# Prefix scan first in both passes of an attention recurrence, and m2 moved ahead of the state's last product

## The chip, the cores and the metric

One core of a Trainium2 chip. The metric is the device time of one execution in microseconds, here the median of several runs. The kernel computes a recurrent attention followed by two expert layers. The change touches the attention alone.

## The reference, cut to what matters

The attention keeps a 40 x 40 state for each of 32 heads (4 batches x 8) over 768 time steps:

```python
for t in range(S):
    y[:, :, t] = einsum('bhd,bhde->bhe', r_t, state)
    Sa = einsum('bhde,bhe->bhd', state, a_t)
    state = state * w_t[:, :, None, :] - einsum('bhd,bhe->bhde', Sa, b_t) \
            + einsum('bhd,bhe->bhde', v_t, k_t)
```

Its output goes through a router that picks one of 8 experts for each token (`_moe_ref`) and a dense layer (`_moe2_ref`). Both stay as they are.

## The kernel before, in words

Time is cut into 12 chunks of 64 steps. The partitions hold two heads in halves of 64, 40 rows of each in use; the free dimension holds 8 slots (`HS`) of 64 times. Two halves of the batch run one after the other, so there are `STEPS` = 24 chunk steps in each pass.

**Decays as scans.** Within a chunk the decay from one time to another is a product of w. VectorE computes it with two `tensor_tensor_scan` operations over one row of 8 x 66 elements (`WIDE` = 66: a pad of zero at either end of each slot): `suffixes` (L433) scans backward and starts at 1, `prefix_starts` (L440) takes the reciprocal of the total into `restart`, `prefixes` (L444) scans forward and starts at 1 / total. `scaled_second` (L452) multiplies b (or k) by the suffixes, `scaled_alpha` (L455) multiplies a by the prefixes. In the second pass `prefixes` also copies the total from `suf` into column 65 of `wq` (L450).

**First pass** (L486 to L505 on VectorE, L685 on ScalarE, L905 on TensorE): for each chunk the products of alpha with second (g1) and the turned second (bt). ScalarE evicts them, SyncE stores g1's blocks to DRAM and loads them again for the inversion, which VectorE does for two groups of chunks and GpSimd for the four others (`invert_blocks`, up to about 292 us). One step runs at the pace of VectorE's five operations. TensorE waits for alpha, the last of them, and SyncE's load of the chunk three ahead into the ring `t_in` waits for it too (`s_alpha1`).

**Second pass** (L512 on VectorE, L745 on ScalarE, L932 on TensorE): one turn for each chunk, and in each turn TensorE works through eighteen groups of 32 small matmuls (`heads`), each of which may wait for an eviction. The order in each engine's queue is written out by hand. The end of a turn on TensorE before the change is: sa's product (L955), sat's product (L956), the part of y from rr and st (L957), the last part of the state (sa with btm, did "st", L959), m2's product (rr with sat, L961), g2's product of the next chunk (L963), `picks` (L965, of the previous chunk's output, waits for `out_of["st"]`), and y's last product (L967, waits for the masked m2). In the trace these groups are, in that order, bank<-w_tm,inv; inv,w_tm; rr,st; sa_tm,btm; rr,sat; alpha,second; pick,yt; m,btm.

ScalarE evicts sa (L758) and then sat (L760). VectorE scales the next state by the total of the *next* chunk (`swt`, L550), taken from column 65 of `wq` and from its crossed copy, and then masks m2 (L554). The crossed copy is made by two DMAs from SyncE, `cross_wq` (L339), in front of the load of t_in (L383), the store of rows (L385) and the loads of vtm, vt, inverses and rr. `y_out` (L458) scales y by the prefixes.

Of the kernel before, what the change touches and what calls it, by code (L numbers as in the profile page):

```python
# [10 lines left out]
ALU = mybir.AluOpType  # L11
# [4 lines left out]
PARTS = 128  # L16
BATCH, HEADS, SEQ, DIM = 4, 8, 768, 40
HALF = PARTS // 2
C = 64
# [141 lines left out]
def attention(nc, inp, dram, keep):  # L161

    with ExitStack() as ctx:
# [32 lines left out]
        def late_part(n, **sizes):  # L196
# [41 lines left out]
        s_set, s_suf, s_rw, s_wq, s_wc, s_second, s_alpha1, s_alpha0, s_alpha = (m_.sem(n) for n in (  # L238
            "s_set", "s_suf", "s_rw", "s_wq", "s_wc", "s_second", "s_alpha1", "s_alpha0", "s_alpha"))
# [31 lines left out]
        def _(sp):  # L271
            def load_t(j):
                if j >= TR:
                    if j - TR < STEPS:
                        sp.wait_ge(s_alpha1, j - TR + 1)
                    elif j - TR == STEPS:
                        sp.wait_ge(s_alpha0, 1)
                    else:
                        sp.wait_ge(s_second, j - TR + 1)
# [59 lines left out]
            def cross_wq(k):  # L339
                sp.wait_ge(s_wc, k + 1)  # L340
                if k >= 3:
                    sp.wait_ge(out_of["y"], k - 1)
# [61 lines left out]
        def _(dve):  # L404
# [4 lines left out]
            dve.memset(restart[:, :, WIDE - 1:WIDE], 1.0).then_inc(s_set, 1)  # L409
# [22 lines left out]

            def suffixes(j):  # L433
                dve.wait_ge(s_t[j % TR], 16 * (j // TR + 1))
# [5 lines left out]
            def prefix_starts(j):  # L440
                dve.wait_ge(s_suf, j + 1)
                dve.reciprocal(restart[:, :, 0:1], suf[j % 2][:, :, 1:2]).then_inc(s_rw, 1)

            def prefixes(j):  # L444
                dve.wait_ge(s_rw, j + 1)
                dve.tensor_tensor_scan(out=forward(wq[j % 3][:, :, :]), data0=forward(w_of(j)), data1=forward(restart[:, :, :]), initial=0.0,
                                       op0=ALU.mult, op1=ALU.add).then_inc(s_wq, 1)
                dve.wait_ge(s_wq, j + 1)
                if j >= STEPS:
                    dve.tensor_copy(wq[j % 3][:, :, WIDE - 1:WIDE], suf[j % 2][:, :, 1:2]).then_inc(s_wc, 1)  # L450

            def scaled_second(j):  # L452
                dve.tensor_tensor(second[:, :, :], in_of(j, 1), suf[j % 2][:, :, 2:WIDE], ALU.mult).then_inc(s_second, 1)

            def scaled_alpha(j, sem):  # L455
                dve.tensor_tensor(alpha[:, :, :], in_of(j, 0), wq[j % 3][:, :, 0:C], ALU.mult).then_inc(sem, 1)  # L456
# [29 lines left out]
            for k in range(STEPS):  # L486
                suffixes(k)
                prefix_starts(k)
                prefixes(k)
                if k >= 1:  # L490
                    dve.wait_ge(did["bt"], k)
# [1105 lines left out]
```

## Time and profile before

| | us |
|---|---|
| median of 3 runs | 1057.15 (1055.74 to 1058.28) |
| the profiled execution | 1054.7 |
| its span | 1052.9 |
| TensorE busy | 952.9 (90%) |
| VectorE busy | 711.5 (68%) |
| ScalarE busy | 442.8 (42%) |
| GpSimd busy | 268.6 (26%) |

Shares over the whole span mix stages with different limits. Attention ends near 373 us; its first pass ends near 133 us. Starts and durations in a timeline are in us from the span's start; the ends of matmuls are modelled, and a group "x32" is one call of `heads`. The time from the start of one group to the start of the next is what the group costs the queue.

### The profile page before, as it was taken

Reading aid. Unit: us, or ns where it says so; the run is one execution under the profiler, and the core shown is the slowest. Engines: PE = TensorE matmul, PEld = TensorE weight load, DVE = VectorE, ACT = ScalarE, POOL = GpSimd, SP = SyncE. Lnnn points to the kernel's source line nnn. Section 1 sums busy time; section 2 is a strip of 40 time slices with the busy share of each in tenths; the row PEclk is TensorE's granted clock in tenths of the full one; section 3 lists DMA queues with packets and bytes.
Section 4 is the critical chain, followed back from the end, with each engine's and each line's share of the span. In section 5 each row is a group of like instructions: output and inputs, shape, how many; then the busy total and the mean of one; then the engine's idle time right before and its main releaser. Section 6 shows DMA issues by size and latency. Waiting matters only on the chain. (4 is left out here: it accounts for less than half of the span.)

```text
span 1052.9 us, 48691 instructions
## 1 busy us (share of the span) xinstructions
PE 952.9 (90%) x21425; PEld 874.8 (83%) x21425; DVE 711.5 (68%) x1076; ACT 442.8 (42%) x940; POOL 268.6 (26%) x348
## 2 busy tenths in 40 slices
PE   3526779999999998999999999879999999999997
PEld 2426769999999958998999999668999999999997
DVE  8997958899988764555555555567666565656664
ACT  5525635755555604545555555513222212222211
POOL 1009989798900003222111100241001000000000
PEclk9999988999999999999999999999999999999999
DMA  7968866898898539998676755120100101010100
GB/s 220 234 173 189 203 140 188 242 246 236 238 243 241 150 119 307 332 294 278 190 249 214 228 169 169 41 79 13 38 1 26 26 1 26 2 26 1 26 1 26
DMA packets 116866, 153.19 MB, mean 145 GB/s; under 512 B 68516, under 2 KB 87860, under 8 KB 116420
## 3 DMA queue, kind: packets, MB, share of 16 engines
q1 hardware_dynamic: 102468, 118.68, 40.3%
q0 software_dynamic: 5872, 25.28, 7.8%
q10 hardware_dynamic: 8464, 8.43, 2.4%
q8 instruction: 36, 0.59, 0.2%
q14 instruction: 26, 0.21, 0.1%
HBM read 126.72 MB, written 19.23 MB: 139 GB/s over the span
## 5 line engine op out<-in xcount | busy, mean ns | idle before, releaser
L1468 ACT CAST g_hi<-g 128x512 fp32r<-128x512 f32 x96 | 59.5, 620 | 278.0 <-DVE g L1412 274.4
L1321 PE MATMUL y_bank<-w_out_hi,g_hi 128*128 128x320 f32 x380 | 119.0, 313 | 5.1 <-DVE g_lo L1386 4.3
L1109 PE MATMUL h_bank<-xt,w 128*128 128x128 f32 x992 | 122.0, 282 | 1.8 <-issue 1.8
L1149 DVE TENSOR_TENSOR w_lo<-w_all,w_hi 128x640 fp32r<-128x640 f32 x124 | 101.7, 826 | 31.9 <-ACT w_hi L1189 27.0
L1109 PEld LDWEIGHTS h_bank<-xt,w 128*128 128x128 f32 x992 | 115.8, 195 | 6.0 <-issue 2.2
L1321 PE MATMUL y_bank<-w_out_hi,g_lo 128*128 128x320 f32 x380 | 118.0, 310 | 0.0
L1321 PE MATMUL y_bank<-w_out_lo,g_hi 128*128 128x320 f32 x380 | 117.9, 310 | 0.0
L1408 DVE TENSOR_SCALAR neg<-h_bank,slope 128x512 f32<-128x512 f32 x96 | 72.0, 750 | 65.8 <-PE h_bank L1308 65.4
L1308 PE MATMUL h_bank<-xt_hi,w_in_hi 128*128 128x512 f32 x288 | 113.1, 393 | 0.5 <-DVE xt_hi L1369 0.5
L1308 PE MATMUL h_bank<-xt_hi,w_in_lo 128*128 128x512 f32 x288 | 112.1, 389 | 0.0
L1386 DVE TENSOR_TENSOR g_lo<-g,g_hi 128x512 fp32r<-128x512 f32 x96 | 66.5, 693 | 65.9 <-ACT g_hi L1468 64.5
L1142 DVE SCALAR_TENSOR_TENSOR ht_lo<-h_bank,ht_hi 128x512 fp32r<-128x512 f32 x62 | 42.8, 692 | 88.6 <-ACT ht_hi L1182 83.7
L1189 ACT CAST w_hi<-w_all 128x640 fp32r x124 | 89.7, 727 | 29.3 <-PE y_bank L1121 20.6
L127 POOL TENSOR_TENSOR solved<-solved,share 128x31 f32<-128x31 f32 (+15 forms) x124 | 99.2, 800 | 9.7
L784 PE MATMUL bank<-alpha,second 40*64 40x64 f32 x1568 | 44.6, 269 | 56.5 <-DVE alpha L456 55.7
L124 POOL TENSOR_TENSOR share<-solved,blk 128x31 f32<-128x31 f32 (+15 forms) x124 | 89.0, 718 | 9.7
L784 PEld LDWEIGHTS bank<-alpha,second 40*64 40x64 f32 x1568 | 38.6, 178 | 59.8 <-issue 59.8
L95 POOL DMA_INDIRECT x<-x_rows_mid,order x31 | 32.1, 1035 | 197.8 <-DVE order L609 97.5
L1321 PEld LDWEIGHTS y_bank<-w_out_hi,g_hi 128*128 128x128 f32 x380 | 71.9, 189 | 10.6 <-DVE g_lo L1386 5.9
L1121 PE MATMUL y_bank<-w_hi,ht_hi 128*128 128x320 f32 x248 | 79.2, 319 | 0.0
L1182 ACT ACTIVATE ht_hi<-h_bank 128x512 fp32r<-128x512 f32 x62 | 37.1, 598 | 97.3 <-PE h_bank L1109 97.3
L1121 PE MATMUL y_bank<-w_lo,ht_hi 128*128 128x320 f32 x248 | 76.7, 309 | 0.0
(213 smaller groups left out, 2145.1 us busy)
## 6 DMA issues: line engine op xcount, KB each, us to landing
w<-w_in SPq DMA_DIRECT2D x31, 1024.0 KB
t_in<-wak_in SPq DMA_DIRECT2D x24, 679.0 KB, 5.7
t_in<-wab_in SPq DMA_DIRECT2D x21, 679.0 KB, 5.0
w_all<-w_in POOLq DMA_DIRECT2D x8, 1280.0 KB, 9.2
rr<-rr_in SPq DMA_DIRECT2D x24, 336.0 KB, 3.5
w_rest<-w_in SPq DMA_DIRECT2D x62, 128.0 KB
vtm<-vtm_in SPq DMA_DIRECT2D x24, 240.0 KB, 3.7
vt<-vt_in SPq DMA_DIRECT2D x24, 224.0 KB, 4.0
```

The lines of the kernel that those rows point to most:

```text
L124: link(eng.tensor_tensor(part, q[:, 0:j + 1, j:j + 1].to_broadcast(shape), h[:, j:j + 1, j + 1:B].to_broadcast(shape), ALU.mult))
L127: link(eng.tensor_tensor(rest, rest, part, ALU.subtract))
L784: last = pe.matmul(out[HALF * to:HALF * to + rows_out, row, n * i:n * i + n], lhs, rhs, start=opens and i == 0, stop=closes and i == HP - 1)
L1109: last = pe.matmul(h_bank[s][h][:, f * ET:(f + 1) * ET], w1[s][:, k, (FH * h + f) * PARTS:(FH * h + f + 1) * PARTS], xt[s][:, k, :], start ...
L1121: last = pe.matmul(y_bank[s][:, 0:FEAT], h[s][:, f, :], w[:, f, :], start=f == 0 and n == 0, stop=f == NF - 1 and n == 2)
L1149: dve.tensor_tensor(piece(w2_lo, p), of_expert(e, p), piece(w2_hi, p).bitcast(F32), ALU.subtract).then_inc(s_w2lo, 1)
L1189: act.copy(piece(w2_hi, p), of_expert(e, p)).then_inc(s_w2hi, 1)
L1308: last = pe.matmul(h_bank[j % 2][:, :], w[:, k, f * PARTS:(f + 1) * PARTS], x_part[b % 2][:, k, :], start=n == 0, stop=n == len(passes) - 1)
L1321: last = pe.matmul(y_bank[n][:, 0:FEAT], g_part[j % RING][:, n * PARTS:(n + 1) * PARTS], v[:, f, :], start=f == 0 and p == 0, stop=f == NF ...
L1386: dve.tensor_tensor(g_lo[j % RING][:, :], g[j % 2][:, :], g_hi[j % RING][:, :].bitcast(F32), ALU.subtract).then_inc(s_glo, 1)
L1408: dve.tensor_scalar(neg[j % 2][:, :], h_bank[j % 2][:, :], 0.0, keep.slope[:, f:f + 1], ALU.min, ALU.mult).then_inc(s_neg, 1)
L1468: act.copy(g_hi[j % RING][:, :], g[j % 2][:, :]).then_inc(s_ghi, 1)
```

## The change

- `prefixes` runs first and starts at 1, so column 64 of `wq` holds the total; `suffix_starts` takes its reciprocal into the other end of `restart`; `suffixes` runs last and starts at 1 / total. The copy of the total into column 65 is gone, and the wait of the second scan on itself with it.
- `scaled_alpha` comes ahead of `scaled_second` in the first pass; TensorE and SyncE's loads wait for `s_second`.
- In the second pass the prefix scan stands where the suffix scan was and the other way round. The state is scaled at the end of a chunk by that chunk's own total.
- `cross_wq(k)` waits for the prefix scan instead of the copy, and for the output of one chunk later, from k = 2 on.
- ScalarE evicts sat ahead of sa. TensorE computes sat ahead of sa, and m2 ahead of the last product of the state. VectorE masks m2 ahead of the scaling of the state.

```diff
--- before.py
+++ after.py
@@ -235,8 +235,8 @@
         s_blk, s_tt = ([[m_.sem(f"{n}{s}_{part}") for part in range(GROUP)] for s in range(3)] for n in ("s_blk", "s_tt"))
         s_ax_vtm, s_vt_rr = (m_.sem(n) for n in ("s_ax_vtm", "s_vt_rr"))
         s_step, s_step_dve = m_.sem("s_step"), m_.sem("s_step_dve")
-        s_set, s_suf, s_rw, s_wq, s_wc, s_second, s_alpha1, s_alpha0, s_alpha = (m_.sem(n) for n in (
-            "s_set", "s_suf", "s_rw", "s_wq", "s_wc", "s_second", "s_alpha1", "s_alpha0", "s_alpha"))
+        s_set, s_suf, s_rw, s_wq, s_second, s_alpha0, s_alpha = (m_.sem(n) for n in (
+            "s_set", "s_suf", "s_rw", "s_wq", "s_second", "s_alpha0", "s_alpha"))
         names = ("turned", "across", "joint", "g1", "bt", "w", "s", "u", "ktm", "z", "m1", "sa", "sat", "st", "g2", "m2", "y", "pick")
         did = {n: m_.sem("pe_" + n) for n in names}
         out_of = {n: m_.sem("ev_" + n) for n in names}
@@ -271,12 +271,7 @@
         def _(sp):
             def load_t(j):
                 if j >= TR:
-                    if j - TR < STEPS:
-                        sp.wait_ge(s_alpha1, j - TR + 1)
-                    elif j - TR == STEPS:
-                        sp.wait_ge(s_alpha0, 1)
-                    else:
-                        sp.wait_ge(s_second, j - TR + 1)
+                    sp.wait_ge(s_second, j - TR + 1)
                 src = inp["wab"][j] if j < STEPS else inp["wak"][j - STEPS]
                 used = slice(0, PARTS if j < TR else USED)
                 sp.dma_start(t_in[j % TR][used, :], src[used]).then_inc(s_t[j % TR], 16)
@@ -337,9 +332,9 @@
                 sp.dma_start(vt[0:USED], inp["vt"][k][0:USED]).then_inc(s_vt_rr, 16)
 
             def cross_wq(k):
-                sp.wait_ge(s_wc, k + 1)
-                if k >= 3:
-                    sp.wait_ge(out_of["y"], k - 1)
+                sp.wait_ge(s_wq, STEPS + k + 1)
+                if k >= 2:
+                    sp.wait_ge(out_of["y"], k)
                 at = wq_both[(STEPS + k) % 3]
                 for h in two:
                     sp.dma_start(at[rows(h), HS:HS + HP, :], at[rows(1 - h), HP:HS, :]).then_inc(s_wqx[k % 2], 16)
@@ -406,7 +401,7 @@
             dve.memset(keep.eye[:, :], 0.0).then_inc(s_ones, 1)
             dve.memset(restart[:, :, :], 0.0).then_inc(s_set, 1)
             dve.wait_ge(s_set, 1)
-            dve.memset(restart[:, :, WIDE - 1:WIDE], 1.0).then_inc(s_set, 1)
+            dve.memset(restart[:, :, 0:1], 1.0).then_inc(s_set, 1)
             dve.memset(swt[:, :, :], 0.0).then_inc(out_of["st"], 1)
             dve.memset(yt[:, :, :], 0.0)
             dve.wait_ge(s_const, 4)
@@ -430,30 +425,30 @@
             def own_and_crossed(k, part):
                 return wq_both[(STEPS + k) % 3][:, :, part].rearrange("q (g p) t -> q g p t", p=HP)[:, 0:3:2]
 
+            def prefixes(j):
+                dve.wait_ge(s_t[j % TR], 16 * (j // TR + 1))
+                if j >= 1:
+                    dve.wait_ge(s_suf, j)
+                dve.tensor_tensor_scan(out=forward(wq[j % 3][:, :, :]), data0=forward(w_of(j)), data1=forward(restart[:, :, :]), initial=0.0,
+                                       op0=ALU.mult, op1=ALU.add).then_inc(s_wq, 1)
+
+            def suffix_starts(j):
+                dve.wait_ge(s_wq, j + 1)
+                dve.reciprocal(restart[:, :, WIDE - 1:WIDE], wq[j % 3][:, :, C:C + 1]).then_inc(s_rw, 1)
+
             def suffixes(j):
-                dve.wait_ge(s_t[j % TR], 16 * (j // TR + 1))
+                dve.wait_ge(s_rw, j + 1)
                 if j >= 2:
                     dve.wait_ge(s_second, j - 1)
                 dve.tensor_tensor_scan(out=backward(suf[j % 2][:, :, :]), data0=backward(w_of(j)), data1=backward(restart[:, :, :]), initial=0.0,
                                        op0=ALU.mult, op1=ALU.add).then_inc(s_suf, 1)
 
-            def prefix_starts(j):
+            def scaled_second(j):
                 dve.wait_ge(s_suf, j + 1)
-                dve.reciprocal(restart[:, :, 0:1], suf[j % 2][:, :, 1:2]).then_inc(s_rw, 1)
-
-            def prefixes(j):
-                dve.wait_ge(s_rw, j + 1)
-                dve.tensor_tensor_scan(out=forward(wq[j % 3][:, :, :]), data0=forward(w_of(j)), data1=forward(restart[:, :, :]), initial=0.0,
-                                       op0=ALU.mult, op1=ALU.add).then_inc(s_wq, 1)
-                dve.wait_ge(s_wq, j + 1)
-                if j >= STEPS:
-                    dve.tensor_copy(wq[j % 3][:, :, WIDE - 1:WIDE], suf[j % 2][:, :, 1:2]).then_inc(s_wc, 1)
-
-            def scaled_second(j):
                 dve.tensor_tensor(second[:, :, :], in_of(j, 1), suf[j % 2][:, :, 2:WIDE], ALU.mult).then_inc(s_second, 1)
 
-            def scaled_alpha(j, sem):
-                dve.tensor_tensor(alpha[:, :, :], in_of(j, 0), wq[j % 3][:, :, 0:C], ALU.mult).then_inc(sem, 1)
+            def scaled_alpha(j):
+                return dve.tensor_tensor(alpha[:, :, :], in_of(j, 0), wq[j % 3][:, :, 0:C], ALU.mult)
 
             def y_out(k):
                 dve.wait_ge(did["y"], k + 1)
@@ -484,30 +479,30 @@
                 return dve.tensor_tensor(by_row(dst), wide(src), later, ALU.mult)
 
             for k in range(STEPS):
+                prefixes(k)
+                suffix_starts(k)
                 suffixes(k)
-                prefix_starts(k)
-                prefixes(k)
                 if k >= 1:
                     dve.wait_ge(did["bt"], k)
+                scaled_alpha(k)
                 scaled_second(k)
-                scaled_alpha(k, s_alpha1)
                 if k == AT_DVE:
                     for g in range(BY_DVE):
                         for part in range(GROUP):
                             dve.wait_ge(s_blk[g][part], 16)
                     dve.wait_ge(s_eye, 2)
                     invert_halves(dve, s_step_dve, blk, solved, share_dve)
+            prefixes(STEPS)
+            suffix_starts(STEPS)
             suffixes(STEPS)
-            prefix_starts(STEPS)
-            prefixes(STEPS)
             dve.wait_ge(did["bt"], STEPS)
+            scaled_alpha(STEPS).then_inc(s_alpha0, 1)
             scaled_second(STEPS)
-            scaled_alpha(STEPS, s_alpha0)
-            suffixes(STEPS + 1)
+            prefixes(STEPS + 1)
+            suffix_starts(STEPS + 1)
             dve.wait_ge(did["g2"], 1)
             masked(g2, BC).then_inc(out_of["g2"], 1)
-            prefix_starts(STEPS + 1)
-            prefixes(STEPS + 1)
+            suffixes(STEPS + 1)
             first_choices = chain(dve, s_choice)
             for k in range(STEPS):
                 more = k + 1 < STEPS
@@ -519,13 +514,15 @@
                         dve.sem_inc(out_of["pick"], 1)
                 dve.wait_ge(did["w"], k + 1)
                 if more:
-                    scaled_alpha(STEPS + k + 1, s_alpha)
+                    scaled_alpha(STEPS + k + 1).then_inc(s_alpha, 1)
                 if k + 2 < STEPS:
-                    suffixes(STEPS + k + 2)
+                    if k >= 1:
+                        dve.wait_ge(out_of["y"], k + 1)
+                    prefixes(STEPS + k + 2)
                 dve.wait_ge(did["m1"], k + 1)
                 masked(m1, BB).then_inc(out_of["m1"], 1)
                 if k + 2 < STEPS:
-                    prefix_starts(STEPS + k + 2)
+                    suffix_starts(STEPS + k + 2)
                 dve.wait_ge(did["z"], k + 1)
                 w_flat = w_tm[:, :, :].rearrange("q (r p) e -> q r (p e)", r=2)
                 dve.tensor_tensor(w_flat, w_flat, BA[:, :, 0:HP * DIM], ALU.add).then_inc(out_of["z"], 1)
@@ -535,23 +532,23 @@
                 else:
                     dve.sem_inc(s_second, 1)
                 if k + 2 < STEPS:
-                    prefixes(STEPS + k + 2)
+                    suffixes(STEPS + k + 2)
                 elif k + 2 == STEPS:
                     dve.wait_ge(s_iota, 8)
                     choices_top(FIRST, first_choices)
                 else:
                     dve.memset(one_hot[:, :, FINAL], 0.0)
                     choices_one(FIRST, first_choices).then_inc(s_hot, 1)
+                dve.wait_ge(did["m2"], k + 1)
+                masked(m2, BA).then_inc(out_of["m2"], 1)
                 dve.wait_ge(did["st"], k + 1)
                 if (k + 1) % NCHUNK == 0:
                     last = dve.memset(swt[:, :, :], 0.0)
                 else:
-                    dve.wait_ge(s_wqx[(k + 1) % 2], 32 * turn(k + 1))
+                    dve.wait_ge(s_wqx[k % 2], 32 * turn(k))
                     last = dve.tensor_tensor(by_row(swt), BD[:, :, 0:HP * DIM].rearrange("q r (p e) -> q r p e", e=DIM),
-                                             own_and_crossed(k + 1, slice(WIDE - 1, WIDE)).to_broadcast([PARTS, 2, HP, DIM]), ALU.mult)
+                                             own_and_crossed(k, slice(C, C + 1)).to_broadcast([PARTS, 2, HP, DIM]), ALU.mult)
                 last.then_inc(out_of["st"], 1)
-                dve.wait_ge(did["m2"], k + 1)
-                masked(m2, BA).then_inc(out_of["m2"], 1)
                 if more:
                     dve.wait_ge(did["g2"], k + 2)
                     masked(g2, BC).then_inc(out_of["g2"], 1)
@@ -754,10 +751,10 @@
                 act.copy(btm[:, :, :].rearrange("q p e -> q (p e)"), btm_all[:, k].rearrange("q p e -> q (p e)"))
                 if k + 1 < STEPS:
                     cross_alpha(k + 1)
+                act.wait_ge(did["sat"], k + 1)
+                act.copy(by_row(sat[:, :, :]), wide(BA)).then_inc(out_of["sat"], 1)
                 act.wait_ge(did["sa"], k + 1)
                 act.copy(flat(sa_tm[:, :, :]), narrow(BC)).then_inc(out_of["sa"], 1)
-                act.wait_ge(did["sat"], k + 1)
-                act.copy(by_row(sat[:, :, :]), wide(BA)).then_inc(out_of["sat"], 1)
                 if k + 1 < STEPS:
                     act.wait_ge(did["z"], k + 1)
                     off_diagonal(k + 1)
@@ -892,7 +889,7 @@
                 return lambda b, p: (across_now[quarter(b), p, :], d1_now[s][quarter(b), p, :])
 
             def g1_product(count):
-                arrive(s_alpha1, count)
+                arrive(s_second, count)
                 arrive(out_of["g1"], count)
                 heads(with_alpha(second), BA, C, done="g1")
 
@@ -925,7 +922,7 @@
                 pe.wait_ge(out_of[n], JOINED + 1)
             pe.wait_ge(out_of["bt"], STEPS + 1)
             warm(2)
-            pe.wait_ge(s_alpha0, 1)
+            pe.wait_ge(s_second, STEPS + 1)
             heads(with_alpha(second), BC, C, done="g2")
             warm(3)
             pe.wait_ge(keep.s_gw, 32)
@@ -952,13 +949,13 @@
                 arrive(out_of["m1"], i)
                 heads(from_k(lambda i, q, m: m1[rows(m), slot(q, i), :]), BB, C, closes=False)
                 arrive(out_of["z"], i)
+                heads(sat_product, BA, C, done="sat")
                 heads(sa_product, BC, DIM, done="sa")
-                heads(sat_product, BA, C, done="sat")
                 heads(from_s(lambda i, q, m: at_m(rr, i, q, m, live(m))), BB, C, opens=False, closes=False)
+                arrive(out_of["sat"], i)
+                heads(m2_product, BA, C, done="m2")
                 arrive(out_of["sa"], i)
                 heads(from_b(lambda i, q, m: sa_tm[rows(m), slot(q ^ m, i), :]), BD, DIM, opens=False, done="st")
-                arrive(out_of["sat"], i)
-                heads(m2_product, BA, C, done="m2")
                 arrive(s_second, i + (STEPS + 1))
                 heads(with_alpha(second), BC, C, done="g2")
                 arrive(out_of["st"], i + 1)
```

## Rows read from the trace of the kernel before

**Rows 1.** The page, busy time of each engine over the span.

```profile
PE 952.9 (90%) x21425; PEld 874.8 (83%) x21425; DVE 711.5 (68%) x1076; ACT 442.8 (42%) x940; POOL 268.6 (26%) x348
```

**Rows 2.** Windows: stretch, busy us of each engine, granted clock, DMA share, GB/s.

```profile
25.00:50.00 25.00, 11.67 (x384) 10.96 (x384) 24.30 (x33) 13.28 (x37) 0.00 (x0) 1.00 0.94 240
...
155.00:160.00 5.00, 5.00 (x200) 4.82 (x196) 2.93 (x4) 1.28 (x3) 4.56 (x6) 0.50 0.90 252
...
200.00:225.00 25.00, 23.99 (x1537) 22.84 (x1539) 23.51 (x36) 16.75 (x44) 23.04 (x26) 1.00 0.92 247
...
300.00:350.00 50.00, 48.31 (x3167) 46.05 (x3157) 42.14 (x72) 28.96 (x71) 0.00 (x0) 1.00 0.88 237
```

**Rows 3.** Timeline of VectorE, one first-pass step: start us, us, engine, line, operation.

```profile
21.50 1.25 DVE L437 TENSOR_TENSOR_SCAN suf<-t_in,restart 128x528 f32<-128x528 f32 x1
...
23.03 1.26 DVE L446 TENSOR_TENSOR_SCAN wq<-t_in,restart 128x528 f32<-128x528 f32 x1
24.32 0.69 DVE L453 TENSOR_TENSOR second<-t_in,suf 128x512 f32<-128x512 f32 x1
...
25.53 1.25 DVE L437 TENSOR_TENSOR_SCAN suf<-t_in,restart 128x528 f32<-128x528 f32 x1
```

**Rows 4.** Timeline of VectorE, a contended turn: a scan, what follows it, the copy.

```profile
171.86 1.69 DVE L437 TENSOR_TENSOR_SCAN suf<-t_in,restart 128x528 f32<-128x528 f32 x1
173.47 0.66 DVE L484 TENSOR_TENSOR m<-bank,later 128x512 f32<-128x512 f32 x1
...
176.80 0.39 DVE L450 COPY wq<-suf 128x8 f32<-128x8 f32 x1
```

**Rows 5.** Timeline of VectorE, first pass, the two long waits for TensorE.

```profile
91.83 0.69 DVE L453 TENSOR_TENSOR second<-t_in,suf 128x512 f32<-128x512 f32 x1 [2.09 <-PE bank L784]
...
100.18 0.89 DVE L453 TENSOR_TENSOR second<-t_in,suf 128x512 f32<-128x512 f32 x1 [3.61 <-PE bank L784]
```

**Rows 6.** Timeline of TensorE, end of a quiet turn (matmul groups).

```profile
314.23 0.66 PE L784 MATMUL bank<-w_tm,inv 64*64 64x40 f32 x32
...
316.13 0.69 PE L784 MATMUL bank<-rr,sat 40*64 40x64 f32 x32
316.62 0.68 PE L784 MATMUL bank<-alpha,second 40*64 40x64 f32 x32
317.08 0.66 PE L846 MATMUL bank<-pick,yt 40*64 40x48 f32 x32
317.72 0.66 PE L784 MATMUL bank<-m,btm 64*40 64x64 f32 x32
```

**Rows 7.** Timeline of VectorE in the same turn.

```profile
316.16 0.49 DVE L550 TENSOR_TENSOR swt<-bank,wq 128x320 f32<-128x320 f32 x1
316.88 0.69 DVE L484 TENSOR_TENSOR m<-bank,later 128x512 f32<-128x512 f32 x1 [0.23 <-PE bank L784]
```

**Rows 8.** Timeline of ScalarE in the same turn.

```profile
314.95 0.43 ACT L758 COPY sa_tm<-bank 128x320 f32<-128x320 f32 x1 [1.95 <-PE bank L784]
315.40 0.59 ACT L760 COPY sat<-bank 128x512 f32<-128x512 f32 x1
```

**Rows 9.** Timeline of TensorE, the contended turn with the longest wait for swt.

```profile
270.31 0.68 PE L784 MATMUL bank<-alpha,second 40*64 40x64 f32 x32
271.18 0.68 PE L846 MATMUL bank<-pick,yt 40*64 40x48 f32 x32 [0.19 <-DVE swt L550]
271.78 0.66 PE L784 MATMUL bank<-m,btm 64*40 64x64 f32 x32
```

**Rows 10.** Timeline of SyncE's DMA issues in a quiet turn.

```profile
309.93 0.59 SPq L282 DMA_DIRECT2D t_in<-wak_in  x1
...
313.57 0.35 SPq L332 DMA_DIRECT2D vtm<-vtm_in  x1
```

**Rows 11.** The tile vtm in the second pass: time from issue to landing.

```profile
DMA to landing us min/median/max: 2.6/3.7/5.0
```

**Rows 12.** Timeline of TensorE, a turn that starts late.

```profile
327.85 0.22 PE L784 MATMUL bank<-swt,alpha 40*64 40x40 f32 x1 [0.39 <-DMA vtm<-vtm_in]
```

## The prediction

> **What bounds the kernel now.** I read four views. The busy shares [rows 1] say only that TensorE is the fullest engine over all stages; the windows [rows 2] cut the span where the change acts. In the first pass (from 5 to 133 us) VectorE is the full engine, 24.30 of 25 us, and TensorE is under half. In the second pass (139 to 373 us, 24 turns of one loop) it is TensorE: 48.31 of 50 us at 300 to 350, where GpSimd is silent, and 23.99 of 25 at 200 to 225, where GpSimd inverts blocks and VectorE too stands at 23.51. After 373 us nothing is touched; what attention gains or loses reaches the end whole. The timelines then give each chain.
>
> **First pass.** One step is 4.03 us (21.50 to 25.53 [rows 3]), VectorE's five operations end to end: scan, reciprocal, scan, two products. The change keeps all five but swaps the scans and the products. What goes is one wait that an operation makes on its own engine's last result. Before, the second scan is followed by a wait on itself and `second` starts 0.03 us after its end (23.03 + 1.26 = 24.29, then 24.32 [rows 3]). After, `scaled_alpha` needs only the older scan and follows the suffix scan without waiting; such a follower starts 0.08 us before the end (171.86 + 1.69 = 173.55, then 173.47 [rows 4]). So 0.11 us a step. `second` waits for the suffix scan, but that ends during the alpha product. TensorE's first product waits for the last product of the step as before, SyncE's load waits for `second` in place of `alpha`, again the last. Of the 25 steps, 23 are bound by VectorE; in two it waits 2.09 and 3.61 us for TensorE [rows 5], and there 0.11 us buys nothing. 23 x 0.11 = **2.5 us less**. DMA engines are busy 0.94 of this stretch [rows 2]; at a period of 3.92 that would be 0.97, near the edge, so the gain may be anything between 0 and 2.5. I take 2.5 because in the uncontended steps like the one shown the scan waits for no load.
>
> The Trainium skill, "VectorE: DVE Perf Modes", § The DRAIN you can't avoid, says that chaining operations with or without a semaphore costs the same. By it the 0.11 us would be 0 and the first pass unchanged. Rows 3 and 4 speak against it: 0.03 us after the end with a wait, 0.08 before the end without.
>
> **The copy of the total.** The copy into `wq` goes in 24 places. In the quiet part of the second pass swt's product starts only with TensorE's release (316.16 us [rows 7]), so the copy is covered. In the contended part it takes 0.39 us ahead of swt [rows 4] and is on the way to the picks in the steps where VectorE is late. What takes its place decides what that is worth, next.
>
> **Second pass, TensorE's new order.** I take the quiet step and count from the start of the product that yields `sa` (314.23 [rows 6]), call it 0. Today the picks start at 2.85 and the product that yields y at 3.49 (317.08, 317.72). The picks need swt, y's product needs the masked m2. Today swt is computed first, well before the picks, and m2's mask (316.88 [rows 7]) is what y's product waits for: mask end 317.57, product 317.72, so 0.15 from VectorE's end to TensorE's start.
>
> After the change:
> - sat's product stands at 0 and lasts 0.66 or so [rows 6]; ScalarE takes it 0.06 later and needs 0.59 [rows 8]; TensorE starts 0.14 after that: m2's product at 1.45, against a bare queue time of 1.35. It starts 1.90 today.
> - m2's product ends at 1.45 + 0.69 = 2.14; VectorE's mask starts 0.06 later, 2.20.
> - The mask holds VectorE for 0.61. swt comes **behind it** on VectorE, at 2.81 at the earliest, though st's product (1.94 + 0.52 = 2.46) was ready. 0.49 for swt [rows 7]: 3.30.
> - The picks, behind their wait for swt, start at 3.44 instead of 2.85. Everything on TensorE's queue waits with them.
> - y's product follows after a bare group spacing of 0.48 (316.13 to 316.62 is 0.49, 316.62 to 317.08 is 0.46 [rows 6]), since m2 is long there: 3.92 instead of 3.49.
>
> So a quiet step becomes **0.43 us longer**. The old wait of 0.15 us for m2 goes, and a new one of 0.59 us for swt comes: the state's last product moved back by a whole product, and swt moved back behind the mask too. Downstream (g2's mask, yt, alpha) VectorE has 0.2 us or more of waiting for TensorE and moves along.
>
> There are 8 quiet turns of 9.0 us. Seven cost 0.43; the last has a memset of 0.33 us in place of swt's product and costs 0.27: 3.3 us.
>
> In the 14 turns between 170 and 300 us GpSimd slows VectorE (a scan takes 1.69 us [rows 4] against 1.25), and the picks wait for swt already today by 0 to 0.41 us; the worst turn goes from 270.31 to 271.18 where 0.46 is bare [rows 9]. By the same groups in the timeline of each, the stretch from sa's product to y's is 3.50 to 3.87 us, in sum 50.5. The new stretch is 3.92 in each (3.76 in the one with a memset) as long as the scan ends before m2's product; in the worst turn it ends 2.26 after 0, so an unwaited mask could start at 2.18, just ahead of the 2.20. Sum 54.7: **4.2 us more**. The two first turns, partly at 0.50 of the full clock [rows 2], follow the same logic, about 0.35 each: 0.7. Second pass: 3.3 + 4.2 + 0.7 = **8.2 us more**.
>
> **Queues behind the moved waits.** SyncE's crossing of wq for turn k+1 now waits for y_out(k-1), about 1.4 us later than today; the 679 KB load of t_in behind it (309.93 [rows 10]) goes out near 311.35. Its own reader is a turn further on, so it is covered. But vtm's load, issued at 313.57, now runs right behind it. It takes 3.7 us, at worst 5.0 [rows 11], and the loop's first product needs it at 318.58: one turn already waits 0.39 us for it [rows 12]. The longer turn gives 0.43 back. Bounds: -0.5 (today's waits for vtm vanish) and +0.4 in half of the turns, +4. I take 0. The wait added on VectorE (prefixes on y_out) is met when it is reached, since y_out stands ahead of it in the same queue.
>
> **Sum.** -2.5 + 8.2 = +5.7 us. The profiled execution took 1054.7 us with a span of 1052.9, so it would take 1060.4. The runs' median is 1057.15, 2.5 above it; **1057.15 + 5.7 = 1062.8 us**.
>
> **Rivals.**
> - *Faster: VectorE's relief wins.* In the contended turns VectorE is nearly full [rows 2]; each turn loses a copy and a wait, 0.39 + 0.11 us, and TensorE's waits for VectorE there, 2.0 us in sum at the picks and 2.3 at the masked m1, could vanish. With the first pass, -2.5 - 4.3: 1050.4. It needs swt no later than today, that is the mask of m2 out of its way; that holds only where the scan ends later than m2's product by the mask's 0.6 us, and no turn shows that. Against it also: alpha's start, which the masked m1 hangs on, waits for TensorE. Chance 0.11.
> - *Cancelled.* The mask finds room while the scan runs late in most contended turns, so that these lose only the 0.05 us of the worst one; 3.3 + 0.7 + 0.7 - 2.5: +2.2 us or less, 1057 to 1059.3. Chance 0.12.
> - *First pass gives nothing* (the page's rule, or DMA at 0.94 binding): +8.2, 1065.4. Chance 0.17.
> - *The later t_in costs vtm's readers*: +1 to +4 on top, 1064 to 1067. Chance 0.12.
> - *The clock.* TensorE runs at half its clock at 155 to 160 us [rows 2] after the first turn's pauses. A stretch of that kind that ends sooner or later would move the time by some us either way, whatever the change does; about 0.04 each way, inside the other cases.
> - *The forecast itself*, 1060 to 1064: 0.48.
>
> Within 0.2% is 1055.0 to 1059.3, about what a measurement of this kernel can tell from no change. Faster 0.11, same 0.12, slower 0.77. The range leaves out the faster rival and a few hundredths above: 1056.5 to 1068.
>
> **What the profile would show.** First-pass period 3.92 us, the alpha product starting 0.08 before the suffix scan's end. In a quiet turn: m2's product at 1.45, its mask at 2.20, swt at 2.81, the picks at 3.44 with VectorE's swt as what TensorE waited for in nearly all turns, no wait for m, a period of 9.44. Wrong if the picks start by 2.9, if the quiet period stays at 9.0, if waits for vtm are many, or if the first pass keeps 4.03.

## The result, and the profile after

The changed kernel takes 1066.87 us in the median of 4 runs (1065.77 to 1069.86), the kernel before 1056.45 (1054.51 to 1058.28, 4 runs): ratio **1.0111, 95% interval 1.0087 to 1.0136**. Beside other kernels on another chip it was 1.0136 (1.0095 to 1.0177). Slower, as forecast, but by 10.4 us where 5.7 were forecast, at the upper edge of the range.

The profiled execution after has a span of 1068.1 us, 15.2 above that before; it was the longest of its four. One profile below, that of e1, is of a slow execution (1064.47 us at a mean granted clock of 0.975; that kernel's fastest took 1048.06), so no size is taken from it. The difference by stage, from the timelines of TensorE (start of a turn = first product of swt with alpha):

| stretch | before, us | after, us | difference | forecast |
|---|---|---|---|---|
| to the start of turn 0 | 139.04 | 136.64 | -2.4 | -2.5 |
| turns 0 and 1 | 30.68 | 32.00 | +1.3 | +0.7 |
| turns 2 to 22 (21 turns) | 194.42 | 208.77 | +14.35 | +7.2 |
| turn 23 and all behind | 688.8 | 690.7 | +1.9 | +0.3 |

The last line is mostly not the change's: that stretch took 683 to 694 us in the fourteen profiles of this study, whatever was done to attention; turns 0 and 1, partly at half the clock, took 27 to 33, so the +1.3 of the second line is inside that spread too (the changed kernel's other profile, e12, has 30.0 us there, 0.7 less than before). Single runs of one kernel spread by 10 us or more, so the size of each term below is read from the timelines. What needs an explanation is the third line. First the end of a quiet turn after the change, TensorE and then VectorE, to be set against [rows 6] and [rows 7]:

```profile
322.83 0.65 PE L781 MATMUL bank<-inv,w_tm 64*40 64x64 f32 x32
323.28 0.65 PE L781 MATMUL bank<-w_tm,inv 64*64 64x40 f32 x32
323.72 0.66 PE L781 MATMUL bank<-rr,st 40*40 40x64 f32 x32
324.26 0.69 PE L781 MATMUL bank<-rr,sat 40*64 40x64 f32 x32
324.75 0.51 PE L781 MATMUL bank<-sa_tm,btm 64*40 64x40 f32 x32
325.19 0.69 PE L781 MATMUL bank<-alpha,second 40*64 40x64 f32 x32
326.25 0.68 PE L843 MATMUL bank<-pick,yt 40*64 40x48 f32 x32 [0.36 <-DVE swt L549]
326.73 0.66 PE L781 MATMUL bank<-m,btm 64*40 64x64 f32 x32
327.68 0.22 PE L781 MATMUL bank<-swt,alpha 40*64 40x40 f32 x1 [0.30 <-issue]
```

```profile
325.02 0.69 DVE L479 TENSOR_TENSOR m<-bank,later 128x512 f32<-128x512 f32 x1 [0.57 <-PE bank L781]
325.62 0.48 DVE L549 TENSOR_TENSOR swt<-bank,wq 128x320 f32<-128x320 f32 x1
```

From sat's product at 322.83: m2's product at 1.43 us, its mask at 2.19, swt at 2.79, the picks at 3.42, y's product at 3.90. The forecast had 1.45, 2.20, 2.81, 3.44 and 3.92. That mechanism is there as it was worked out, in nearly every turn. Three things were not worked out. The first is the last row: the next turn starts 0.95 us after y's product. Before, from the last row of [rows 6] at 317.72 to this one, it was 0.86:

```profile
318.58 0.22 PE L784 MATMUL bank<-swt,alpha 40*64 40x40 f32 x1 [0.20 <-issue]
```

The second is in the list of what TensorE waited for, all turns from the third on (operation waited with, us in total, times, longest):

```profile
PE bank L843 <- DVE swt L549: 7.3, 20, 0.4
...
PE bank L781 <- DMA rr<-rr_in: 3.3, 5, 1.3
PE bank L781 <- DMA vtm<-vtm_in: 3.0, 6, 0.9
```

and the same list of before:

```profile
PE bank L784 <- DVE m L484: 0.9, 4, 0.3
PE bank L784 <- DMA vtm<-vtm_in: 0.8, 2, 0.4
PE bank L846 <- DVE swt L550: 0.2, 1, 0.2
```

The waits for swt were forecast. The waits for two loads, 6.3 us of idle TensorE against 0.8, were not. One of them in the timeline, m1's product held 0.66 us for the load of rr and vt:

```profile
339.46 0.68 PE L781 MATMUL bank<-w_tm,inv 64*64 64x40 f32 x32
340.80 0.69 PE L781 MATMUL bank<-rr,vt 40*64 40x64 f32 x32 [0.66 <-DMA rr<-rr_in]
```

SyncE's issues show where these loads come from; in [rows 10] t_in went out 3.64 us ahead of vtm, now it is 2.37:

```profile
318.66 1.11 SPq L340 DMA_DIRECT2D wq<-wq  x2
319.81 0.61 SPq L277 DMA_DIRECT2D t_in<-wak_in  x1
...
322.18 0.35 SPq L327 DMA_DIRECT2D vtm<-vtm_in  x1
...
325.01 0.33 SPq L322 DMA_DIRECT2D rr<-rr_in  x1
```

Counted from the start of the turn, t_in goes out at 1.67 us in the median, 0.33 before: 1.3 us later. vtm goes out at the same 4.0 us, but its landing went from 3.7 us (median, [rows 11]) to 4.8.

The third is TensorE's clock. In turn 6 of the changed kernel (turns are counted from 0) TensorE waited 0.93 us for vtm and then 1.32 for rr, and behind the second wait the granted clock fell to its lower level, 0.50 (1.2 GHz of 2.4), for 3.4 us. The two waits and the clock before, in and behind that stretch:

```profile
208.37 0.22 PE L781 MATMUL bank<-swt,alpha 40*64 40x40 f32 x1 [0.93 <-DMA vtm<-vtm_in]
...
212.13 0.69 PE L781 MATMUL bank<-rr,vt 40*64 40x64 f32 x32 [1.32 <-DMA rr<-rr_in]
```

```profile
207.50:213.70 6.20, 4.02 (x260) 3.86 (x261) 4.39 (x6) 2.60 (x7) 5.65 (x8) 1.00 0.95 218
213.70:217.10 3.40, 3.40 (x148) 3.40 (x148) 2.75 (x3) 0.67 (x2) 3.17 (x4) 0.50 0.97 262
217.10:221.00 3.90, 3.24 (x205) 2.98 (x201) 2.19 (x4) 3.76 (x11) 3.51 (x6) 1.00 0.61 152
```

The late products of that turn took 4.75 us where the turns around it took 3.9. In turns 2 to 22 of the kernel before the clock was 1.00 throughout.

To compare kernels I add up, over turns 2 to 22, from the starts of TensorE's groups: the **order** stretch (first late product to y's product), the time of u's group over its bare 0.57 us (**held for rr and vt**), the **gap** from y's product to the next turn at its smallest, what its sum has above that (mostly **held for vtm**), and how long the clock was at its **lower level** in these turns. One profile stands behind each row; the two of the changed kernel agree within 0.7 us over the 21 turns, and so do those of e5 and e6. All in us:

| kernel | 21 turns | order stretch, mean | held for rr, vt | smallest gap | above it | lower clock |
|---|---|---|---|---|---|---|
| before | 194.4 | 3.57 | 0.6 | 0.85 | 0.7 | 0 |
| changed | 208.8 | 3.94 | 4.9 | 0.95 | 1.5 | 3.4 |
| changed, again (e12) | 208.1 | 3.92 | 4.8 | 0.95 | 0.7 | 3.4 |
| order only (e2) | 203.6 | 3.99 | 0.0 | 0.95 | 0.4 | 0 |
| late load only (e11) | 204.3 | 3.66 | 7.2 | 0.85 | 2.8 | 6.8 |
| scans and late load (e1) | 206.9 | 3.62 | 6.4 | 0.85 | 5.7 | 13.7 |
| changed, swt ahead (e4) | 206.2 | 3.78 | 5.2 | 0.85 | 3.0 | 6.8 |
| changed, load first (e3) | 201.4 | 3.90 | 0.0 | 0.95 | 0.4 | 0 |
| changed, three semaphores (e8) | 202.2 | 3.90 | 0.0 | 0.95 | 0.4 | 0 |
| scans, load first (e5) | 195.8 | 3.50 | 5.3 | 0.85 | 0.8 | 0 |
| e5 and a wait in the first pass (e6) | 195.8 | 3.51 | 3.6 | 0.85 | 1.4 | 0 |
| scans, three semaphores (e7) | 192.5 | 3.50 | 1.6 | 0.85 | 1.0 | 0 |
| e7, sat first (e9) | 196.7 | 3.67 | 1.7 | 0.85 | 0.5 | 0 |
| e7, m2 first (e10) | 206.1 | 4.21 | 0.0 | 0.85 | 0.4 | 0 |

So the 14.35 us of the changed kernel are 21 x 0.37 = 7.7 of order, 4.3 held for rr and vt, 0.8 for vtm, 21 x 0.10 = 2.1 of gap, and -0.5 of the rest. About 0.8 of the 7.7 is the one turn at the lower clock: where the changed order runs with its loads in time (e3, e8) it is 6.9.

The last column goes with the late load. In each of the five profiles that have it (changed, e12, e11, e1, e4) the clock fell in these turns, each time behind waits for vtm or rr in the same turn (0.34 and 1.13 us in e12; 0.74 and 1.21, then 0.51 and 1.37 in e11; 0.52 and 1.14, then 2.11 in e1; 1.84 in e4); in the other nine it never fell. Such waits don't always bring it: in turn 4 of e5 TensorE waited 0.34 and then 1.36 us, and the clock stayed at 1.00.

### The profile page after: what moved, and what is told of

The parts are those of the page before. It is cut to its first block and busy times, and to the rows that moved or that the text cites. A ratio compares the mean times of both kernels' runs of the same rounds, so it can differ in the third digit from the quotient of the medians.

```text
span 1068.1 us, 48716 instructions
## 1 busy us (share of the span) xinstructions
PE 953.7 (89%) x21425; PEld 876.1 (82%) x21425; DVE 701.3 (66%) x1052; ACT 440.6 (41%) x940; POOL 265.8 (25%) x348
## 5 line engine op out<-in xcount | busy, mean ns | idle before, releaser
L127 POOL TENSOR_TENSOR solved<-solved,share 128x31 f32<-128x31 f32 (+15 forms) x124 | 95.6, 771 | 9.7
## 6 DMA issues: line engine op xcount, KB each, us to landing
w_all<-w_in POOLq DMA_DIRECT2D x8, 1280.0 KB, 10.2
```

Source lines behind the costliest of these rows:

```text
L127: link(eng.tensor_tensor(rest, rest, part, ALU.subtract))
```

## The experiments

Theory A: the new order makes the picks late. Theory C: the crossing of wq, and with it the load of t_in, go out later, and that costs TensorE waits for the loads behind it. Rival B to A: the late load is what costs, the order little.

**e2, the order alone.** The kernel before with only the swaps on TensorE, ScalarE and VectorE:

```diff
+                heads(sat_product, BA, C, done="sat")
                 heads(sa_product, BC, DIM, done="sa")
-                heads(sat_product, BA, C, done="sat")
...
+                arrive(out_of["sat"], i)
+                heads(m2_product, BA, C, done="m2")
                 arrive(out_of["sa"], i)
...
-                arrive(out_of["sat"], i)
-                heads(m2_product, BA, C, done="m2")
```

> The kernel before with only the new order at the end of a turn (sat ahead of sa, m2 ahead of the state's last product, m2's mask ahead of swt). Scans, copy and SyncE's waits are those of before. Theory A: picks at 3.44 us after the turn's first late product, sum 8 to 10 us on top of before, 1064 to 1067, and no more waits for rr and vtm than before. Rival B: under 3 us on top of before.

Measured: ratio 1.0072 (1.0038 to 1.0106), 1058.36 us beside 1050.48 for the kernel before on that chip. The 21 turns take 9.1 us more, the loads hold nobody. Theory A holds. The order stretch gives 8.8 of the 9.1 us, more than the 7.2 forecast; what is more lies in the contended turns (up to 4.29 us, against 3.89 in the quiet ones). The gap gives 2.1, and 1.8 comes back, half of it from the loads that hold nobody now.

**e1, all but the order.** The changed kernel with the four swaps undone.

> The changed kernel with the old order at the end of a turn: sa ahead of sat on TensorE and ScalarE, the state's last product ahead of m2, swt ahead of m2's mask. The scans, the missing copy and SyncE's later waits stay. Theory A (the order costs the time: picks 0.59 us late in each turn): the turn's end returns to 3.49 us from sa's product to y's, so 9 us less than the changed kernel's 1067, 1054 to 1058. Rival B (the later load of t_in costs most): waits for rr and vtm stay, and the time stays above 1061.

Measured: ratio 1.0052 (1.0011 to 1.0093), 1058.07 us beside 1050.48. The order stretch is back (3.62), and yet the 21 turns took 206.9 us. In the profiled execution TensorE waited 6.9 us for vtm and 4.4 for rr, and behind the longest of these waits, 2.1 us, the clock was at its lower level from 285.9 to 296.1 us, so the 12.5 us over before are no measure of the late load:

```profile
PE bank L781 <- DMA vtm<-vtm_in: 6.9, 8, 2.1
PE bank L781 <- DMA rr<-rr_in: 4.4, 8, 1.1
```

The expected 1054 to 1058 was counted from a kernel before of 1056.45; beside the 1050.48 of this chip it is 1048 to 1052. Theory A fell as the whole cause: what is left without the order costs too.

**e11, the late load alone.** The kernel before with one condition changed:

```diff
-                if k >= 3:
-                    sp.wait_ge(out_of["y"], k - 1)
+                if k >= 2:
+                    sp.wait_ge(out_of["y"], k)
```

> The kernel before with one line changed: the crossing of wq waits for the output of one chunk later, as in the change, so that it and the load of t_in behind it go out some 1.4 us later. Theory C (the late load costs by itself, and more where the turn is short): waits for vtm and rr of 8 us or more in the 21 turns from turn 2, which take over 202 us in place of 194.4; 6 to 10 us slower than before. Rival (the late load hurts only beside the new order or the new scans): under 197 us for these turns and no measurable change.

Measured: ratio 1.0080 (1.0048 to 1.0112), and in the turns 9.9 us more, of which 6.6 are waits for rr and vt and 2.1 for vtm; another 2.2 us are the order stretches of the two turns at the lower clock (4.69 and 4.48 where 3.50 is usual). The waits of TensorE:

```profile
PE bank L784 <- DMA rr<-rr_in: 5.3, 9, 1.4
PE bank L784 <- DMA vtm<-vtm_in: 4.0, 8, 0.7
```

vtm's load takes 4.7 us to land instead of 3.7:

```profile
DMA to landing us min/median/max: 2.6/4.7/5.6
```

One condition on SyncE costs 9.9 us in the turns where the whole change costs 14.35. With the changed order the same late load costs less, 6.5 to 7.4 us by e8 and e3 below; that this is because each turn is longer already is my reading.

**e3 and e8, the changed kernel with the load in time.** e3 puts the load ahead of the crossing:

```diff
-                if more:
-                    cross_wq(k + 1)
                 if k + TR < STEPS:
                     load_t(STEPS + k + TR)
+                if more:
+                    cross_wq(k + 1)
```

> The changed kernel with SyncE's load of t_in issued ahead of the crossing of wq, so that it no longer stands behind the wait for y_out. Theory C (the later load is what came on top of the forecast): the waits for rr and vtm, 6.3 us in sum, go back to under 1.5, and the time falls by 4 to 6 us to 1061 to 1063. Rival: these waits come from the longer turn itself or from the crossing, and the time stays within 1 us of 1067.

e8 gives the crossings three semaphores in turn instead of two. With two, the crossing of chunk k+1 must not count up a semaphore on which y_out(k-1) still waits; with three, it only has to wait for y_out(k-2), as before the change:

```diff
+        s_wqx = [m_.sem(f"s_wqx{s}") for s in range(3)]
...
-                if k >= 2:
-                    sp.wait_ge(out_of["y"], k)
+                if k >= 3:
+                    sp.wait_ge(out_of["y"], k - 1)
...
-                    dve.wait_ge(s_wqx[k % 2], 32 * turn(k))
+                    dve.wait_ge(s_wqx[k % 3], 32 * turn(k, 3))
```

> The changed kernel whole, with three semaphores for the crossings, so that crossing and load go out where they did before. Theory C (late load): turns as in the run with the load ahead of the crossing, 201 us from turn 2 to the last (changed kernel: 208.8), no wait for rr or vtm; 6 to 7 us under the changed kernel. Rival (it was the crossing, or having the load ahead of everything, that helped there): 205 us or more.

Measured: e3 1.0070 (1.0030 to 1.0109), e8 1.0075 (1.0042 to 1.0109); 201.4 and 202.2 us for the 21 turns, 7.4 and 6.5 less than the changed kernel, and no wait for a load in either, nor a lower clock. Both agree with theory C: 5 of these us are the time held for rr and vt, about 1 that for vtm, 0.8 the slow late products of turn 6. The totals say less. e3 was expected 4.6 to 6.6 us over the kernel before and came 8.9 over the one on its chip, and both intervals overlap that of the changed kernel. What is left over before, 7.0 and 7.8 us, is the order with its gap less what the scans give (against e7, which has the scans and the old order, e8 takes 9.7 us more). e8's list of waits holds these and no load:

```profile
PE bank L844 <- DVE swt L550: 6.9, 19, 0.4
...
PE bank L782 <- DVE m L480: 0.8, 3, 0.3
```

**e4, swt ahead of the mask on VectorE,** the rest as changed.

> The changed kernel with swt ahead of m2's mask on VectorE; TensorE's order stays new. If VectorE's queue (the mask in front of swt) is half of the delay, swt starts 2.52 us after the first late product and the picks at 3.16 instead of 3.43; y's product then waits for the mask, 3.75 instead of 3.91: 3 to 4 us less in sum, 1063 to 1064. If only TensorE's order matters, no change from 1067.

Measured: 1.0087 (1.0052 to 1.0122). In a quiet turn:

```profile
338.61 0.64 PE L781 MATMUL bank<-inv,w_tm 64*40 64x64 f32 x32
...
341.75 0.68 PE L843 MATMUL bank<-pick,yt 40*64 40x48 f32 x32
342.35 0.66 PE L781 MATMUL bank<-m,btm 64*40 64x64 f32 x32
```

The picks start 3.14 us after the first late product and y's product 3.74, as expected (3.16, 3.75). So of the 0.57 us by which the picks came late, 0.28 was VectorE's queue (the mask in front of swt) and the rest TensorE's (the state's last product moved back). The order stretch falls by 0.16 us a turn. 3 to 4 us less were expected; the 21 turns take 2.6 less, and the total shows no clear gain. Waits for vtm grow (3.0 above the smallest gap), and behind one of them, 1.84 us, the clock was at its lower level for 6.8 us: that turn took 12.1 us where 9.3 is usual.

**e9 and e10, the two swaps one by one,** on the kernel of e7 below.

> The kernel with the scans and three semaphores, and of the new order only sat ahead of sa (TensorE and ScalarE). Expected in a quiet turn: the state's last product at 1.81 us after the first late product instead of 1.35 (it waits for sa's copy behind sat's), picks at 3.2, y's product at 3.85. It also tells whether the longer gap at the loop's end (0.95 instead of 0.86 us) comes with this swap.

> The kernel with the scans and three semaphores, and of the new order only m2's product ahead of the state's last product, with sa still ahead of sat and swt ahead of the mask. Expected in a quiet turn: m2 waits for sat's copy, 1.90 instead of 1.35; picks at 3.6, y's product at 4.2, as far behind as the mask waits for swt. It also tells whether the longer gap at the loop's end comes with this swap.

e9: a single run, 1053.31 us. The group ahead of the state's last product takes 0.87 us where 0.45 is bare, and 0.22 of the 0.43 comes back behind it, since m2's product is no longer held for sat's copy. y's product comes at 3.67 in the mean, not 3.85: 0.17 us a turn over e7. e10: a single run, 1061.96 us, m2's product held for sat's copy (the group ahead of it takes 1.00), y's product at 4.21, as expected. Moving m2 ahead is the dear part, unless sat goes ahead too. Neither alone shows the gap of 0.95.

**The gap.** The smallest gap is 0.95 us in the kernels where y's product is not held for m2's mask (changed, e2, e3, e8, e12) and 0.85 in all where it is (before, e1, e4, e5, e6, e7, e9, e10, e11). So of the 0.15 us that the old wait for m2 cost in front of y's product, 0.10 had been covering something at the loop's end that is now bare. That the sequencer catches up during that wait is my reading; it was not tested by itself.

**e5 and e6, the scans, and a wait that isn't needed.** e5 is e1 with the load first. e6 adds one line to it, in the first pass:

```diff
                 if k >= 1:
                     dve.wait_ge(did["bt"], k)
+                dve.wait_ge(s_suf, k + 1)
                 scaled_alpha(k)
```

> The scans of the change (prefix first, no copy), the old order at the end of a turn, and the load of t_in ahead of the crossing. If the scans and the missing copy are worth what the rows say: 3.3 us in the first pass (0.15 us in 22 steps) and up to 2 us in the turns in which GpSimd is busy: 1051 to 1053, faster than before by 0.4%. If the scans bring nothing outside the first pass: 1053 to 1054.

> The same kernel with one wait added in each first-pass step: the alpha product waits for the suffix scan in front of it on the same engine, which it doesn't need. If such a wait costs a start at the end of the scan instead of before it: 0.11 to 0.15 us in each of some 22 steps, 2.5 to 3.4 us more than the kernel without it. By the page of the Trainium skill on VectorE, where a semaphore between two operations costs nothing: no difference.

Measured: e5 0.9991 (0.9963 to 1.0018), e6 1.0010 (0.9977 to 1.0044). The totals can't tell them apart; the timelines of VectorE can. e5 and then e6, a first-pass step:

```profile
22.49 1.26 DVE L443 TENSOR_TENSOR_SCAN suf<-t_in,restart 128x528 f32<-128x528 f32 x1
23.66 0.67 DVE L451 TENSOR_TENSOR alpha<-t_in,wq 128x512 f32<-128x512 f32 x1
...
24.85 1.25 DVE L432 TENSOR_TENSOR_SCAN wq<-t_in,restart 128x528 f32<-128x528 f32 x1
```

```profile
23.22 1.26 DVE L443 TENSOR_TENSOR_SCAN suf<-t_in,restart 128x528 f32<-128x528 f32 x1
24.58 0.69 DVE L451 TENSOR_TENSOR alpha<-t_in,wq 128x512 f32<-128x512 f32 x1
...
25.80 1.25 DVE L432 TENSOR_TENSOR_SCAN wq<-t_in,restart 128x528 f32<-128x528 f32 x1
```

Without the wait the alpha product starts 1.17 us after the scan, with it 1.36, and the step takes 3.89 against 4.10 us in each of the first steps. The Trainium skill, "VectorE: DVE Perf Modes", § The DRAIN you can't avoid, says of eight copies in a row that a semaphore after each costs nothing extra. Here one costs 0.2 us behind a scan of 1.26, so the measurement decides against it for this pair of operations.

Where GpSimd is active the same wait costs nothing. The periods of the steps from about 105 us on are 5.27, 5.33, 5.27, 5.21, 5.03 us in e6 and 5.28, 5.33, 5.25, 5.17, 5.03 in e5. The alpha product starts 0.10 to 0.11 us after the scan's end in the one and 0.07 to 0.09 before it in the other, but it then lasts 0.83 to 0.89 against 1.03 to 1.10 us.

e5 missed its 1051 to 1053: with the load *ahead* of everything, m1's product was held 4.0 us for rr in three of the early turns:

```profile
PE bank L781 <- DMA rr<-rr_in: 4.0, 3, 1.6
```

Earlier is not simply better either. Beside the new order, whose turns are longer, the same placing caused no wait (e3).

**e7, the best of it.** The scans of the change, the old order, and the three semaphores, so that crossing and load go out as before.

> The scans of the change, the old order at the end of a turn, and three semaphores for the crossings of wq in place of two, so that a crossing (and the load of t_in behind it) needs no wait for the newest y_out and goes out where it did before. If the late load was the whole extra cost and the scans bring what the first pass showed: waits for rr and vtm as before (u's group 0.57 to 0.60 us a turn), 24 turns in no more time than before (second turn to last under 194 us), 2 us less at the end of the first pass, and a time 0.2 to 0.5% under that of before. Rival: the scans disturb the loads in another way, and the waits stay.

Measured: 1050.82 us beside 1054.78, ratio **0.9945 (0.9917 to 0.9973)**: faster than the kernel before, by 0.5%. The 21 turns take 192.5 us; the picks never wait for swt (mean spacing 0.47 us against 0.56 before).

**e12** is the changed kernel once more, beside e11.

> The changed kernel as it is, beside the run above on the same chip: by the first measurement 1.1% over the kernel before, with 3 to 7 us of waits for rr and vtm in the 21 turns from turn 2. It shows how far these waits repeat from one execution to another.

Measured: ratio 1.0136 (1.0095 to 1.0177). Its waits repeat: 3.2 us for rr and 1.9 for vtm, and in turn 6 the clock fell for 3.4 us again, behind waits of 0.34 and 1.13 us.

## Why the forecast was half right

**The order, 8.2 us forecast.** Right in mechanism and nearly in size. Each number of the quiet turn came within 0.02 us. In 21 turns it was 7.7 us against 7.2, of which about 0.8 belongs to the lower clock of one turn. The 0.7 for the first two turns can't be judged: +1.3 in one profile, -0.7 in the other. That the picks wait for VectorE's swt in nearly every turn shows (20 times, 7.3 us of idle time), and there is no wait for the masked m2 any more.

**"... and +0.4 in half of the turns, +4. I take 0."** This is the step that failed, the term of the sum for the queues behind the moved waits. The forecast saw that t_in would go out 1.4 us later and that vtm ran behind it, then reasoned from one load and its median landing time. The runs show 5.1 us held for loads in the 21 turns, and it was mostly the other one: rr and vt, which m1's product needs, 4.3 us. Putting the load back in time takes 6.5 (e8) to 7.4 us (e3) out of the changed kernel, the lower clock behind the waits included, so that is what the term measured where 0 was taken. e11 shows it in the kernel before: 9.9 us. The queue as a whole had to be weighed: DMA engines 0.88 busy there [rows 2], and t_in and six more transfers in one queue behind a wait that now ends 1.3 us later in a turn of 9 us. By which of them the delay reaches rr and vt no run takes apart. The rival for it was there, with 0.12 and a price of 1 to 4; the price was too low. The rival on the clock took such a stretch for independent of the change; here it came with the waits for loads.

The 5.7 us forecast, the late load and the gap below make 14 to 15 us. That fits the changed kernel beside e11 (14.7 us between medians) and the two profiled executions (15.2), and is above the 10.4 of the first medians, whose interval reaches to 14.4.

**The gap, not in the forecast.** "The old wait of 0.15 us for m2 goes" was counted as a full gain inside the 3.92. 0.10 of it came back at the loop's end, 2.1 us in 21 turns; a quiet turn that no load holds takes 9.50 us, not 9.44. Why it comes back is open.

**First pass, -2.5 forecast, -2.4 found at the start of turn 0,** by other parts than written, so that the two agree is partly luck. The quiet steps gave 0.14 us, not 0.11 (3.89 against 4.03; 15 steps, 2.1 us). The six steps in which GpSimd is active gave nothing: alpha starts earlier, but takes longer:

```profile
107.31 1.36 DVE L443 TENSOR_TENSOR_SCAN suf<-t_in,restart 128x528 f32<-128x528 f32 x1
108.60 1.06 DVE L451 TENSOR_TENSOR alpha<-t_in,wq 128x512 f32<-128x512 f32 x1
```

The product that follows the scan lasts 1.06 us here, against 0.95 in the kernel before at the same place. What the missing wait gave, the slower operation took; e6 against e5 shows the same with nothing else changed. A little came back at the first loads of the second pass, where TensorE waited 0.38 us for ax and not 0.77.

**The copy.** Covered in quiet turns, as forecast; in contended ones it did stand ahead of the picks. With the old order and without it (e7) the picks' spacing falls from 0.56 to 0.47 us, 1.9 us in 21 turns. The scans changed places in e7 too, and no run takes the copy out alone, so that the copy is what gave this is not shown. The changed order gives it away.

## What to carry to other kernels

When a step moves one wait on a DMA queue, weigh every transfer behind it, not the one nearest: with the DMA engines 0.9 busy, a load that went out 1.3 us later made TensorE wait for other loads, 6 to 10 us in 21 turns, and a third semaphore removed that. Such waits can bring TensorE's lower clock behind them, so look at the granted clock of each turn before a longer turn is put down to anything else. When an operation moves ahead of another on two engines, follow the result that the *next* stage waits for: here the state, not m2, was what the picks needed. And a short wait in front of a loop's end may cover the loop's own overhead, so that its removal gives back less than its length.

## What the runs showed of the hardware

- An operation of VectorE that waits for the one before it on the same engine starts 0.10 us after that one's end (e6, where another wait stands in front of it) or 0.03 (before); one that doesn't starts 0.09 us before the end. In quiet steps that makes 0.14 (before against changed) to 0.21 us (e6 against e5) a wait.
- With GpSimd active, a product that starts 0.2 us earlier behind a scan lasts 0.2 us longer (1.03 to 1.10 us in e5, 0.83 to 0.89 in e6), and the step's period stays the same.
- A load in a queue took about 1 us longer to land (vtm 3.7 us before, 4.7 in e11, 4.8 in the changed kernel, medians) when a 679 KB load ahead of it was issued 1.3 to 1.4 us later in a period of 9 to 10 us; with that load in time it took 3.1 (e8).
- In all five profiles with the late load, and in none of the nine others, the granted clock fell to 0.50 in turns 2 to 22: for 3.4 us (changed, e12), twice 3.4 (e11), 6.8 (e4), 3.4 and 10.2 (e1), each time behind one or two waits for loads in the same turn. In e5 it stayed at 1.00 behind waits of 0.34 and 1.36 us.
